# Attention and a gated mixer on one core: keys come by feature, value block sums move to TensorE, and each group's low half is formed one group later

## The reference

```
k_sum = k.reshape(B, H, S/32, 32, D).max(axis=3)        # B=2, H=8, S=768, D=64
v_sum = v.reshape(B, H, S/32, 32, D).mean(axis=3)
local = q k^T / 8 where |i-j| < 16, else -1e9;  coarse = q k_sum^T / 8 + log(32)
a     = softmax([local, coarse]) ;  x = a @ [v, v_sum]
h     = relu(x w_in); u, v = halves of h; v = layer norm(v)
x     = (u * (w_spatial v + b)) w_out
h     = relu(x w_in2); x = (h * sigmoid(conv3(h))) w_out2
```

## Time and profile before

| | |
|---|---|
| median of three runs | 367.46 us (366.86 to 370.37) |
| profiled execution: own time, span | 368.71 us, 366.9 us |
| PE busy | 338.2 us, 92% of the span |
| DVE, ACT, POOL busy | 213.1, 127.0, 115.5 us |
| mean granted TensorE clock | 0.94 of 2.4 GHz |
| first scores, first dense fill, first product of batch 1 | 8.50, 69.59, 124.46 us |
| read from HBM | 27.01 MB |

### The profile page before, as it was taken

How to read it: one execution, slowest core, us unless ns; L and a number is a source line. 1 busy time by engine, 2 the same in 40 slices (tenths; PEclk the granted TensorE clock), 3 DMA queues, 4 the chain that set the end, 5 groups by cost and what they waited for, 6 DMA issues and landing times.

```text
span 366.9 us, 5885 instructions
## 1 busy us (share of the span) xinstructions
PE 338.2 (92%) x2288; PEld 295.8 (81%) x2288; DVE 213.1 (58%) x498; ACT 127.0 (35%) x364; POOL 115.5 (31%) x116
## 2 busy tenths in 40 slices
PE   4577685998998999999999999999999999999996
PEld 4355464676788889988999999999999888889984
DVE  1757576445330599235444697588855667756662
ACT  1555756655652414334211112422312213221111
POOL 3477767654230699960000591000000000000000
PEclk9557858699999999999999999999999999999999
DMA  7996885464000121015400010000000003000004
GB/s 307 324 330 207 277 277 166 125 217 145 2 3 0 45 100 43 2 41 185 119 0 2 4 54 2 1 2 0 0 2 0 0 2 145 27 2 0 2 1 172
DMA packets 9275, 30.53 MB, mean 83 GB/s; under 512 B 1184, under 2 KB 1184, under 8 KB 9248
## 3 DMA queue, kind: packets, MB, share of 16 engines
q1 hardware_dynamic: 9104, 29.77, 24.1%
q10 hardware_dynamic: 144, 0.39, 0.3%
HBM read 27.01 MB, written 3.15 MB: 82 GB/s over the span
## 4 chain that ended last, share of the span: by engine, by line
PE 79%; ACT 8%; DMA 5%; DVE 4%; issue 3%; POOL 0%; DVEq 0%; POOLq 0%
PE bank L756 25%; PE bank L758 25%; PE bank L757 24%; ACT P L470 6%; DMA kw<-in_kw 4%; PE bank L748 2%; PE bank L735 2%; ACT pT L465 1%; DVE P L601 1%; DVE x_l L577 1%; ACT x_h L459 1%; PE bank L725 1%; DVE rinv L584 1%; DMA out<-obuf 1%; DVE ks L541 1%
## 5 line engine op out<-in xcount | busy, mean ns | idle before, releaser
L470 ACT ACTIVATE P<-P,nmax 128x120 f32<-128x120 f32 x96 | 36.7, 383 | 38.7 <-DVE nmax L601 38.7
L758 PE MATMUL bank<-g_h,W_l 128*128 128x384 f32 x128 | 43.0, 336 | 0.0
L757 PE MATMUL bank<-g_l,W_h 128*128 128x384 f32 x128 | 42.9, 335 | 0.0
L756 PE MATMUL bank<-g_h,W_h 128*128 128x384 f32 x128 | 42.9, 335 | 0.0
L577 DVE TENSOR_TENSOR x_l<-bank,x_h 128x256 fp32r<-128x256 f32 x24 | 10.2, 425 | 52.1 <-ACT x_h L459 52.1
L757 PE MATMUL bank<-wo_l,hg_h 128*128 128x512 f32 x96 | 38.0, 396 | 0.0
L758 PE MATMUL bank<-wo_h,hg_l 128*128 128x512 f32 x96 | 38.0, 396 | 0.0
L756 PE MATMUL bank<-wo_h,hg_h 128*128 128x512 f32 x96 | 37.9, 395 | 0.0
L383 POOL TENSOR_TENSOR P<-P,rinv 128x480 f32<-128x480 f32 x24 | 23.7, 987 | 42.0 <-DVE rinv L586 42.0
L758 PE MATMUL bank<-wsT_h,vn_l 128*128 128x384 f32 x96 | 32.1, 334 | 0.0
L756 PE MATMUL bank<-wsT_h,vn_h 128*128 128x384 f32 x96 | 32.1, 334 | 0.0
(11 more groups left out here) (96 smaller groups left out, 778.0 us busy)
## 6 DMA issues: line engine op xcount, KB each, us to landing
kw<-in_kw SPq DMA_DIRECT2D x8, 720.0 KB, 4.3
vw<-in_vw SPq DMA_DIRECT2D x8, 576.0 KB, 5.3
vT<-in_vT SPq DMA_DIRECT2D x8, 384.0 KB, 6.4
out<-obuf SPq DMA_DIRECT2D x12, 256.0 KB, 2.1
qT<-in_q SPq DMA_DIRECT2D x7, 384.0 KB, 5.1
stage<-in_wsT SPq DMA_DIRECT2D x6, 384.0 KB, 2.8
stage<-in_w_in SPq DMA_DIRECT2D x4, 512.0 KB, 10.8
stage<-in_w SPq DMA_DIRECT2D x4, 512.0 KB, 4.9
```

The source lines that it names most:

```text
L470: a.activation(P[:, i % NP_, j, :], P[:, i % NP_, j, :], ACT.Exp, bias=nmax[:, c:c + 1], scale=-1.0, accum_out=rsum[:, c:c + 1]).then_inc( ...
L756: t_.matmul(dst, lhs[0](c), rhs[0](c), start=first, stop=False)
L757: t_.matmul(dst, lhs[0](c), rhs[1](c), start=False, stop=False)
L758: ins = t_.matmul(dst, lhs[1](c), rhs[0](c), start=False, stop=last)
```

## The change

- **Keys.** The host gives the keys by feature without windows (384 KB a pair, `kT`). The windows are copied on the chip from an overlapping view of `kT`: by ACT for the first pair, by POOL for the others (1152 columns, L385 of the new kernel).
- **Block sums.** No `vT` and no `value_sums`. PE makes the sums from the value windows with a 0/1 matrix (`asel`, 96 x 32): 12 products of 128 columns, three accumulated on each of four strips of 32 partitions (fill `vs`); ACT copies them out; one more product with `psel` puts them on the 24 partitions (fill `vp`), one slot later. ACT copies again and SP spreads them with a transfer inside SBUF (`load_sums`) instead of POOL.
- **Order.** `x_l` of a group moves to the slot after its `x_h`, with two banks for the result instead of one (`OT`), so the fills keep banks 0 and 1. DVE takes two of three copies of transposed probabilities, ACT one. PE runs a slot's fills before the transposes instead of behind them. The dense fills start in slot 17 instead of 16, and there is one more slot. POOL takes one split part per slot, two from slot 17 on.
- **Start.** 20 transposes of the identity instead of 16 ahead of the first scores; the first transfers are k, q, v of pair 0, then of pair 1, all on SP; POOL also builds `asel` and `psel`.

```diff
@@ order of work @@
-    WARM = 16
-    SLOTS = NG + 4
+    QB = 3 * BLOCK // 16
+    WARM = 20
+    SLOTS = NG + 5
...
-            fills_at[max(1, GP * p)].append(("vs", p))
+            fills_at[max(0, GP * p - 1)].append(("vs", p))
+            fills_at[max(1, GP * p)].append(("vp", p))
...
-        for n, i in enumerate((16, 17, 18, 19, 20, 21, 22, 23, 24, 24, 25, 25, 26, 27)):
+        for n, i in enumerate((17, 18, 19, 20, 21, 22, 23, 24, 24, 25, 25, 26, 27, 28)):
...
-            return n % 4 if n < ATT else (4 + n - ATT) % 8
+            return n % 2 if n < ATT else (2 + n - ATT) % 8
@@ SP @@
+            def load_sums(p):
+                sp.wait_ge(vsum_ready, p + 1)
+                if p >= NVB:
+                    sp.wait_ge(pv_done, GP * (p - NVB + 1))
+                sp.dma_start(vw[KW:KA, p % NVB, :, :],
+                             vsum[KW:KA, p % 2, :].unsqueeze(1).to_broadcast([NB, NT, 2 * D])).then_inc(vw_ready[p % 2], 16)
@@ POOL @@
+            def spread_windows(p):
+                pool.wait_ge(k_in[p % 2], 16 * (p // 2 + 1))
+                if p >= 2:
+                    pool.wait_ge(qk_done, GP * (p - 1))
+                g.tensor_copy(kw[:, p % 2, :, 0:KW], windows(p)).then_inc(win_pool, 1)
...
+                for _ in range(0 if i < 3 else 1 if i < 17 else 2):
+                    if parts:
+                        split_part(*parts.pop(0))
@@ DVE @@
-                if 3 <= i < NG + 3 and (i - 3) % GP == 0:
+                if 3 <= i < NG + 3 and (i - 3) % GP != 1:
...
+                if i % GP == 1 and i // GP + 1 < NP:
+                    key_maxima(i // GP + 1)
-                if i >= 4:
-                    n = i - 4
+                if i >= 5:
+                    n = i - 5
@@ PE @@
-                if i >= 1:
-                    pe.wait_ge(xl_ready, i)
+                if i >= 2:
+                    pe.wait_ge(xl_ready, i - 1)
...
-                    ins = t_.matmul(bk[KW:KA, 0:2 * D], vb[:, u[1] % 2, :], ident[:, :], start=True, stop=True)
+                    for i in range(3):
+                        for jq in range(4):
+                            ins = t_.matmul(bk[32 * jq:32 * jq + 32, 0:2 * D], asel[:, i, :],
+                                            vw[0:KW, u[1] % NVB, 3 * jq + i, :], start=(i == 0), stop=(i == 2))
+                elif what == "vp":
+                    ins = t_.matmul(bk[KW:KA, 0:2 * D], psel[:, :, :].rearrange("p j m -> p (j m)"), vs_s[:, u[1] % 2, :],
+                                    start=True, stop=True)
...
+                for u in fills_at[i]:
+                    dense(u)
                 if 2 <= i < NG + 2:
                     transpose_probs(i - 2)
-                for u in fills_at[i]:
-                    dense(u)
```

More of the change, by code:

```diff
@@ L138, in attention_mixer_program @@
         bank = [ctx.enter_context(nc.psum_tensor(f"bank{i}", [128, 512], fp32)) for i in range(8)]
-        SC, PTB, OT = bank[4:6], bank[6], bank[7]
+        SC, PTB, OT = bank[4:6], bank[6], [bank[3], bank[7]]
         k_in = [sem(f"k_in{i}") for i in range(2)]
         q_in = [sem(f"q_in{i}") for i in range(2)]
-        vT_at = [sem(f"vT_at{i}") for i in range(2)]
         v_in = [sem(f"v_in{i}") for i in range(NVB)]
@@ L146, in attention_mixer_program @@
         b_in, cw_in = sem("b_in"), sem("cw_in")
[L147 to L150, removed]
+        pool_set, kpads, mask_ready, identf_ready, asel_ready, psel_ready, eps_ready = (
+            sem("pool_set"), sem("kpads"), sem("mask_ready"), sem("identf_ready"), sem("asel_ready"),
+            sem("psel_ready"), sem("eps_ready"))
+        ring_done, ks_ready, win_act, win_pool, kw_ready, vs_ready, vsum_ready = (
+            sem("ring_done"), sem("ks_ready"), sem("win_act"), sem("win_pool"), sem("kw_ready"), sem("vs_ready"),
+            sem("vsum_ready"))
+        vw_ready = [sem(f"vw_ready{i}") for i in range(2)]
         qk_done, max_ready, exp_done, den_ready, rinv_ready, norm_done = (
@@ L233, in gate_out_wait, with windows @@
                 eng.wait_ge(s5_step, G + 1 - G // GC)
+        def windows(p):
+            row = kT[:, p % 2, :]
+            return bass.AP(row.tensor, row.offset, [row.ap[0], [TQ, NT], [1, KW]])
         block = ctx.enter_context(nc.Block())
@@ L288, in _ @@
                 load_v(p)
+                load_sums(p - 1)
                 if n < 6:
@@ L291, in _ @@
                     n += 1
+            load_sums(NP - 1)
+            sp.dma_start(cw[:, :], cw_in2).then_inc(cw_in, 16)
             while n < len(items):
@@ L363, in spread_keys @@
                               ks[:, p % 2, :].unsqueeze(1).to_broadcast([128, NT, NB])).then_inc(kw_ready, 1)
[L365 to L375, removed]
+            def spread_windows(p):
[3 more added lines that the diff above has]
+                g.tensor_copy(kw[:, p % 2, :, 0:KW], windows(p)).then_inc(win_pool, 1)
             parts = [(x, part) for x in items[:KC + KC // 2] for part in range(3)]
             spread_keys(0)
+            in_turn(g.memset(asel[:, :, :], 1.0 / BLOCK))
+            for n, (base, cm, pat) in enumerate([
+                    (-WINDOW, 1, [[64, 3], [-32, 32]]), (WINDOW + BLOCK - 1, -1, [[-64, 3], [32, 32]]),
+                    (-WINDOW, 1, [[0, 3], [0, 32]]), (KW - WINDOW - 1, -1, [[0, 3], [0, 32]])]):
+                ins = g.affine_select(out=asel[:, :, :], in_=asel[:, :, :], compare_op=ALU.is_ge, fill=0.0,
+                                      base=base, pattern=pat, channel_multiplier=cm)
+                if n < 3:
+                    in_turn(ins)
+            ins.then_inc(asel_ready, 1)
+            pool.wait_ge(asel_ready, 1)
+            in_turn(g.memset(psel[:, :, :], 0.0))
+            g.affine_select(out=psel[:, :, :], in_=psel[:, :, :], compare_op=ALU.not_equal, fill=1.0, base=0,
+                            pattern=[[-32, 4], [-1, QB]], channel_multiplier=1).then_inc(psel_ready, 1)
             for i in range(1, NG + 1):
@@ L384, in _ @@
                                 op=ALU.mult).then_inc(norm_done, 1)
+                if i % GP == 1 and i // GP + 1 < NP:
+                    spread_windows(i // GP + 1)
                 if i % GP == 2 and i // GP + 1 < NP:
                     spread_keys(i // GP + 1)
[L387 to L394, removed]
+                for _ in range(0 if i < 3 else 1 if i < 17 else 2):
+                    if parts:
+                        split_part(*parts.pop(0))
             for x in parts:
@@ L425, in _ @@
             a = nc.scalar
-            act.dma_start(qT[:, 0, :], qT_in[0]).then_inc(q_in[0], 16)
             act.wait_ge(eps_ready, 1)
             a.activation(warm[:, :], eps[:, :], ACT.Exp)
+            act.wait_ge(k_in[0], 16)
+            act.wait_ge(kpads, 2)
+            a.activation(kw[:, 0, :, 0:KW], windows(0), ACT.Copy).then_inc(win_act, 1)
             def out_of_ring(u):
@@ L437, in take @@
                 if u[0] == "vs":
+                    a.activation(vs_s[:, u[1] % 2, :], src[:, 0:2 * D], ACT.Copy).then_inc(vs_ready, 1)
+                elif u[0] == "vp":
                     p = u[1]
                     if p >= 2:
-                        act.wait_ge(vw_ready, p - 1)
-                    a.activation(vsum[KW:KA, p % 2, :], src[KW:KA, 0:2 * D], ACT.Copy,
-                                 scale=1.0 / BLOCK).then_inc(vsum_ready, 1)
+                        act.wait_ge(vw_ready[p % 2], 16 * (p // 2))
+                    a.activation(vsum[KW:KA, p % 2, :], src[KW:KA, 0:2 * D], ACT.Copy).then_inc(vsum_ready, 1)
                 elif u[0] == "W":
@@ L458, in _ @@
                     c0 = r * GT * TQ
-                    a.activation(x_h[p // PPB][:, p % PPB, c0:c0 + GT * TQ], OT[:, 0:GT * TQ], ACT.Copy).then_inc(xh_ready, 1)
-                if 3 <= i < NG + 3 and (i - 3) % GP > 0:
+                    a.activation(x_h[p // PPB][:, p % PPB, c0:c0 + GT * TQ], OT[n % 2][:, 0:GT * TQ],
+                                 ACT.Copy).then_inc(xh_ready, 1)
+                if 3 <= i < NG + 3 and (i - 3) % GP == 1:
                     n = i - 3
@@ L763, in dense @@
                 if what == "vs":
-                    pe.wait_ge(vb_ready, u[1] + 1)
+                    pe.wait_ge(v_in[u[1] % NVB], 16 * (u[1] // NVB + 1))
+                    pe.wait_ge(asel_ready, 1)
+                elif what == "vp":
+                    pe.wait_ge(vs_ready, u[1] + 1)
+                    pe.wait_ge(psel_ready, 1)
                 elif u == ("v", 0, 0):
```

77 lines of the change are left out of this document (31 added, 46 removed).

## The result

| | before | changed | forecast |
|---|---|---|---|
| median, us | 367.21 (366.86 to 370.37, 4 runs) | 356.99 (353.28 to 358.0, 4 runs) | 353 (346 to 361) |
| ratio to before, 95% interval | 1 | 0.9685 (0.9595 to 0.9774) | 0.961 |
| span of the profiled run | 366.9 | 356.2 | 352.3 |
| maxima of group 4 / 6 / 16 start | 25.00 / 31.61 / 70.17 | 21.01 / 30.51 / 59.95 | 18.5 / 24.8 / 56.3 |
| first dense fill | 69.59 | 63.28 | 58.8 |

The kernel got faster, by 10.2 us where 14 were forecast. The changed kernel was timed again later beside other kernels: 358.06 us, ratio 0.9739 (0.9717 to 0.9762). I compare experiments that were timed together, and treat a difference of 1 to 2 us between ones that were not as not measured. Medians are over all runs; the ratios, and the costs in us read for experiment 3, leave out a run that is over 1.5% above the fastest of its kernel.

What follows compares the result with a forecast made beforehand. Serial ACT-DVE hand-overs were taken to bound the slots before the dense fills, PE those behind. Saving 10.8 us before the first dense fill and 3.8 after gave 14.6 off 366.9, 352.3; stated as 353 against the median, range 346 to 361.

Steps and rivals of the forecast that it cites:

- rival A: Slots before dense fills: POOL holds `rinv` for most of an instruction each time, 3.6 us a slot, 358 us; chance 0.15.
- What bounds the kernel: Before the dense fills: serial ACT-DVE hand-overs, 2.25 us of a 3.73 us slot, with no engine full.
- Pace of groups 5 to 16: Steady slots: 2.95 us at full clock, a fifth at 4.0 with PE at 1.2 GHz, giving 3.15 a slot.
- The hold by POOL: Steady slots: `rinv` on DVE waits for POOL's current instruction, between nothing and 0.6 us a slot, taken as 0.3.
- POOL's sum of 8.1 per round: Steady slots: POOL's work totals 8.1 us per three slots, 2.7 a slot, making it the fullest engine.
- Block sums on PE: Sums of value windows: 12 products on four strips take 1.6 us at 1.2 GHz, 1.0 at 2.4.
- Rival D: Block sums: strips do not overlap and the clock stays at 1.2 GHz, 6.0 us a slot, 388 us; chance 0.04.
- Groups 1 to 4: Start: groups 1 to 3 at 9.6, 12.1, 14.6 us; group 4 at 18.5 after a 1 to 1.5 us key stall.
- the transfer of the sums: Moved from POOL to SP: costed at nothing beyond a stall of 1 to 1.5 us for pair 2's keys.
- Dense slots: After the first dense fill: 1.3 us for fewer scores and values, 3.5 of PE waits, 1.0 added; net 3.8 saved.
- B: Slots before dense fills: PE stays at 1.2 GHz, 4.0 us a slot, 364 us; chance 0.09.
- C: Slots before dense fills: clock holds and POOL's 2.7 sets the pace, 2.75 us a slot, 348 us; chance 0.17.

Runs made afterwards that it cites:

- experiment 3: Changed kernel with `x_l` formed again in the same slot as `x_h`, the two result banks kept: 361.96 us, ratio 0.9825 to the kernel before.
- 8: Kernel before with only the late `x_l` added (second result bank, extra slot): 361.1 us, ratio 0.9828 to the kernel before.
- run 5: Changed kernel with four idle identity transposes ahead of the transposes in slots 1 to 16: 355.81 us, ratio 0.9681 to the kernel before.
- 2: Changed kernel without the add of 1e-9 ahead of DVE's reciprocal: 354.52 us, ratio 0.9622 to the kernel before.
- 7: Changed kernel with pair 2's loads ahead of pair 0's sums, no add before the reciprocal, four idle transposes a slot: 354.99 us, ratio 0.9611.
- 6: Changed kernel with pair 2's loads ahead of pair 0's sums and no add before the reciprocal: 354.06 us, ratio 0.959 to the kernel before.
- run 1: Changed kernel with pair 2's keys and values loaded ahead of the transfer of pair 0's sums: 356.18 us, ratio 0.9679 to the kernel before.

## Why the prediction was right, and where it was off

- **The number: in the range, and partly by errors that cancel.** 356.99 and 358.06 lie inside 346 to 361, but outside the 350 to 356 that had most of the chances, and at rival A's 358, whose mechanism did not set it. In the profiled run group 4 was 2.5 us late, the two slots behind it took 3.2 more than forecast, the next ten 2.1 less, the step from group 16 to the first dense fill 3.3 instead of 2.5, and the rest saved 0.6 more: 3.9 in all.
- **What bounds the kernel: right.** The serial hand-over between ACT and DVE was the largest single part; 8 (alone, 6.6 us) and 3 (undone, 3.5 to 4.5 us) show it.
- **Pace of groups 5 to 16: right in sum.** Forecast 3.15 (2.95 at the full clock), measured 2.94 over the last ten; over all twelve, with the wait for pair 2's values in the second, 3.24. The hold by POOL was taken as 0.3 a slot; in these ten slots the mean of L604 was 0.44 against 0.16 free, 0.28 more, and leaving out the add gave 0.26 a slot. The granted clock of 0.91 means the lower level for 18% of these slots, near the fifth that was forecast, but its price of 0.2 a slot did not show: run 5, at 0.99, took 0.05 a slot less. Rival A's price, 3.6 a slot, was not reached. The Trainium skill (SBUF — State Buffer, section Who interferes with whom) says that a `tensor_scalar` can contend with POOL and that the later of the two blocks fully; the trace agrees, 0.77 us held to POOL's end. POOL's sum of 8.1 per round was measured as 7.5 (24.85 busy in ten slots): the instructions take what the sum took them at, but the records of neighbours overlap by some 0.06 us (a product of 0.99 at 41.83, the next copy at 42.76).
- **Block sums on PE: right.** 0.86 us at 2.4 GHz and 1.51 at 1.2, forecast 1.0 and 1.6: the four strips do overlap. Rival D falls with it, and so does any large price for changing the mode of the array.

```profile
35.70 0.86 PE L804 MATMUL bank<-vw,asel 96*32 96x128 f32 x24
```

- **Groups 1 to 4: the step that was off.** The first scores came at 5.68, better than the 6.2 forecast, and the keys landed by 3.96. But group 1 waited for pair 1's keys until 9.93 and PE for pair 0's values until 8.86, where I had costed both transfers at nothing. Group 4 came at 21.01 against 18.5. I did foresee pair 2's keys behind the sums (landed 19.8, forecast 17), but stopped there: the same queue also holds pair 2's values, PE's block sums need them one slot later, ahead of the transposes, and group 6 came at 30.51 instead of 24.8. That is 5.7 us late, of which the better pace gave 2.1 back by group 16. The sentence on the transfer of the sums, "I cost it at nothing beyond the stall above", is the one that failed: the stall it meant was that of the keys alone. Some of the 2.5 us at group 4 varies from run to run: in run 3, with the same start, the first waits were shorter and group 4 came at 19.67.
- **Dense slots: right.** 4.4 us saved from the first fill to the end, 3.8 forecast. Of the 3.5 us of waits none stayed.
- **B, C.** PE did not stay at 1.2 GHz. C's pace of 2.75 needs the hold gone: runs 2 and 7 have it, with 2.7.

Open: how much of the start is order and how much bytes. Up to 28 us the transfers run at 190 to 370 GB/s when they run at all; the landing of pair 0's values went from 7.8 to 10.0 us over the ten profiled runs with the same first transfers. That could account for part of the spread of 353 to 358: the two that landed first (3 and 7) were the fastest of their kernels' runs by 2.6 and 3.1 us. It was not tried apart, and it also means that times of early groups in single traces compare only to some 2 us. Also open is whether the clock can cost more at one place: in the profiled run of 6 (357.99 us, the slowest of its runs) PE went to 1.2 GHz at about 57.5 us, ahead of a wait of 1.79 for values, met the first dense products there at 61.90 and came back at about 64.2,

```profile
60.00:64.00 4.00, 3.54 (x29) 2.71 (x30) 0.00 (x0) 0.97 (x5) 3.66 (x5) 0.50 0.43 147
```

while the ones with idle transposes met them at 2.4 GHz, as did the changed kernel without them (1.00 from 63.28 on).

## What to carry to other kernels

When work moves onto the engine whose queue everyone else reads from, its inputs become that queue's waits: follow each transfer that the moved work needs to its issue, past everything that stands ahead of it in the issuing queue, and do so for the first few rounds one by one, since steady rounds hide it. A stall removed from a stretch that is short of bytes can show up at the next transfer, as in run 1; ask what the faster loop will have to wait for before counting the gain. A tiny operation between two engines' large ones can cost far more than its own work if it has to wait for another engine's instruction to end.

## What the runs showed of the hardware that was not expected

A DVE reciprocal of 128 x 4 reading SBUF took 165 to 179 ns in all 24 cases with POOL busy 94% of the time, while an add with a constant on the same 128 x 4 went from 0.16 up to 1.07 us. Both are small single-input operations; only the add was held.
